# Gate logits taken from the attention's output products, head by head, in a one-core kernel of attention and two expert layers

## The chip, the core and the metric

The kernel runs on one core of a Trainium2 chip. The metric is device time in microseconds of one execution, lower is better; the profile of one execution gives every instruction's start and length. Five engines work side by side: PE (matrix products, with its weight loads shown as PEld), DVE (vector), ACT (activation), POOL, and SP, which here only issues DMAs. Each runs its own list of instructions in order and waits on semaphores.

## What is computed

Three layers follow each other (2 batches, 8 heads, 768 positions, head size 64):

```
q_assign, k_assign = argmax cosine with 16 centroids per head
scores = q k^T / 8, masked where q_assign != k_assign
attn   = softmax(scores) v                              # per batch and head
x      = attn as 1536 tokens x 512 (8 heads x 64)
logits = x @ w_gate                                     # 1536 x 8
tokens go to the 8 experts greedily by descending logit, 192 to each
h      = relu(x[mask] @ w1[e]) @ w2[e]
out    = sum over 4 experts of p[:, e] * relu(h @ v1[e]) @ v2[e]
```

## The kernel before, in words

**Attention** runs over 16 pairs (head, batch), numbered n = 2h + b, in a software pipeline. A "turn" works on pair n (now), n + 1 (soon) and n + 2 (later) at once, and the order of the work of each engine in a turn is written out by hand (the functions `turn` of `block.scalar`, `block.vector` and `block.tensor`). Turns of heads 1 to 6 run in a hardware loop, 12 turns in all; the others are unrolled. Each turn ends two half outputs (u = 0, 1), of three 128-row tiles each.

A half output goes like this. PE multiplies v with the probabilities (`values`, L1334 and L1335). The rows of v are kept as a high and a low part beside each other, so the result `ps_o` has 128 partitions: 64 of the high part, 64 of the low part, by 384 positions. ACT copies it to `oT` (`take_oT`, L716). PE turns it back, three transposes with the identity (`tr_out`, L1353), into the shared bank `ps_m`: 128 positions by 128 columns, high and low beside each other. ACT copies the low columns to `o_low` (`take_low`, L724). DVE adds high and low into `o_sum` (L993) and multiplies by the reciprocal of the softmax sum into `X` (L997, `rows_out`). That product counts up `x_done`, and PE's next use of `ps_m`, the transposes of q and k rows for the later pair (`tr_rows`, L1267), waits for it (L1256, L1264).

**Gate.** After the last of 32 half outputs PE goes through the 12 token tiles (L1397 to L1411): four transposes of `X` with the identity (L1402), ACT copies the result to `xT_tile` (L768), four products of it with `gate_w` (128 columns, of which 8 hold the gate's weights, L1409) into bank 2 of `ps_y`. DVE copies the logits of all tiles (L1046). At the same time SP stores `X` to DRAM in one DMA (L394, 3 MB, 12 KB in a row for each partition and batch); its semaphore is `x_stored`.

**Routing.** Eight phases choose an expert each by a search over the bits of the best logits: DVE compares (L1103), PE counts (L1515), DVE decides. The first phases have no other PE work; `keep_running` (L1501) sends products of no use, to keep PE going. From the end of phase 1 on, PE's expert products (`products`, L1442 and L1457) fill the waits. When an expert's tokens are known, POOL gathers their rows from DRAM (`expert_rows`, L581; before the first it waits for `x_stored`, L604), and SP loads the expert's weights (`expert_weights`, L402 and L405).

**Second layer.** 16 rounds of Strassen-like products in split precision, with their weights loaded by L431 and L438.

**Order of the queues around the change.** SP: centroids (L354), gate weights (L356, after a wait for DVE's clearing of `gate_w`), q, k, v of the first two pairs (L362), `domain_probs` (L379), then the loads and moves of every pair; after them the store of `X`, the store of the normalized `domain_probs` (L420) and the experts' weights. DVE: clears (L898), centroid norms (from L910; they wait for both small loads), attention, the normalization of `domain_probs` (L1040 to L1043), the logits.

## Time and profile before

| what | value |
|---|---|
| median of 3 runs | 1087.37 us (1085.91 to 1087.64) |
| the profiled execution's own time | 1086.81 us |
| its span, first to last instruction | 1085.0 us |
| PE busy | 1024.5 us, 94% of the span |
| DVE busy | 623.0 us, 57% |
| ACT busy | 506.3 us, 47% |
| POOL busy | 441.9 us, 41% |

How to read it: busy shares are averages over stages with different limits, so a change in one stage is read from that stage's own rows. In the view of the instructions in order, a row gives start, length, engine, line, operation, output and inputs, and in brackets how long the engine had been idle and what ended it. Matmuls are pipelined: a row's length is more than its share of PE, and the pace is the distance of starts. The chain is the chain of work that ended last, followed back: each of its pieces holds up the end. A granted clock of 1.00 is PE's full 2.4 GHz, 0.50 is 1.2 GHz.

### The profile page before, as it was taken

What the parts mean: (1) busy time and instruction counts of PE and PEld (TensorE: products, weight loads), DVE (VectorE), ACT (ScalarE), POOL (GpSimd) and SP (SyncE); (2) the same over time, 40 slices, a digit from 0 to 9 for tenths busy, and PEclk for the clock granted to TensorE, in tenths of its full rate; (3) what the DMA queues carried; (4) which work ended last, traced back from release to release, by engine and by line L of the source; (5) the groups of instructions that cost most, each with busy time, mean ns of one, the idle gap of its engine ahead of it and who ended that gap; (6) DMA issues with size and microseconds to landing.
All of it is one profiled execution on the core that took longest, in us unless ns stands there. A gap on an engine that the chain in (4) does not pass through costs nothing.

```text
span 1085.0 us, 18093 instructions
## 1 busy us (share of the span) xinstructions
PE 1024.5 (94%) x6458; PEld 934.0 (86%) x6458; DVE 623.0 (57%) x1332; ACT 506.3 (47%) x1007; POOL 441.9 (41%) x363
## 2 busy tenths in 40 slices
PE   3999999999987799999999999999999999999996
PEld 3888888888877789999899988899999888999995
DVE  2788888888835535555223444555559445555542
ACT  3798888888851233333643333233324332333230
POOL 7032323233100111111266685665566756665542
PEclk9999999999997599999999999999999999999999
DMA  3323232332120724445962212211222322212201
GB/s 97 81 74 82 73 80 75 78 81 71 29 118 14 249 79 170 171 171 171 252 167 78 68 49 78 79 61 60 75 78 70 106 78 79 65 59 72 78 1 59
DMA packets 75170, 99.61 MB, mean 92 GB/s; under 512 B 5728, under 2 KB 44640, under 8 KB 74848
## 3 DMA queue, kind: packets, MB, share of 16 engines
q1 hardware_dynamic: 72400, 92.39, 28.0%
q0 software_dynamic: 2704, 6.33, 1.9%
q8 instruction: 43, 0.70, 0.3%
q14 instruction: 23, 0.19, 0.1%
HBM read 79.80 MB, written 6.32 MB: 79 GB/s over the span
## 4 chain that ended last, share of the span: by engine, by line
PE 83%; ACT 9%; DVE 3%; issue 3%; DMA 1%; POOL 1%; ACTq 0%; SPq 0%; DVEq 0%; POOLq 0%
PE ps_y L1416 9%; PE ps_y L1417 9%; PE ps_y L1415 9%; PE ps_h L1442 8%; PE ps_y L1457 7%; PE ps_h L1417 6%; PE ps_h L1415 6%; PE ps_h L1416 6%; PE ps_t L1320 4%; PE ps_s L1307 3%; ACT p_hi L707 2%; PE ps_s L1308 2%; PE ps_m L1281 2%; PE ps_o L1334 2%; PE ps_o L1335 2%
## 5 line engine op out<-in xcount | busy, mean ns | idle before, releaser
L560 POOL TENSOR_TENSOR w_lo<-w_sum,w_hi 128x1792 fp32r<-128x1792 f32 x32 | 129.8, 4079 | 62.8 <-ACT w_hi L782 62.8
L1417 PE MATMUL ps_y<-b_lo,h_hi 128*128 128x512 f32 x384 | 149.7, 390 | 0.0
L1416 PE MATMUL ps_y<-b_hi,h_lo 128*128 128x512 f32 x384 | 149.7, 390 | 0.0
L1415 PE MATMUL ps_y<-b_hi,h_hi 128*128 128x512 f32 x384 | 149.4, 389 | 0.0
L1231 DVE SCALAR_TENSOR_TENSOR Y<-ps_y,mix_n,Y 128x512 f32<-128x512 f32 x84 | 63.0, 750 | 134.5 <-PE ps_y L1417 134.4
L1415 PE MATMUL ps_h<-x_hi,w_hi 128*128 128x384 f32 x384 | 128.6, 335 | 0.0
L1417 PE MATMUL ps_h<-x_lo,w_hi 128*128 128x384 f32 x384 | 128.5, 335 | 0.0
L1416 PE MATMUL ps_h<-x_hi,w_lo 128*128 128x384 f32 x384 | 128.4, 334 | 0.0
L566 POOL TENSOR_TENSOR b_lo<-b_raw,b_hi 128x2048 fp32r<-128x2048 f32 x16 | 74.0, 4626 | 114.4 <-ACT b_hi L789 113.7
L975 DVE TENSOR_TENSOR p_lo<-ps_t,p_hi 128x384 fp32r<-128x384 f32 x192 | 101.6, 549 | 22.5 <-ACT p_hi L707 22.3
L581 POOL DMA_INDIRECT rows_in<-x_rows,ids x16 | 16.7, 1044 | 222.9 <-DVE ids L1083 212.7
L707 ACT CAST p_hi<-ps_t 128x384 fp32r<-128x384 f32 x192 | 87.2, 485 | 37.4 <-PE ps_t L1320 36.1
L966 DVE TENSOR_REDUCE neg_max<-ps_s 128x1 f32<-128x768 f32 x96 | 91.5, 953 | 18.0 <-PE ps_s L1308 17.9
L795 ACT COPY c<-ps_h 128x384 f32<-128x384 f32 x32 | 15.3, 478 | 179.7 <-PE ps_h L1417 179.7
L801 ACT ACTIVATE h_hi<-ps_h 128x384 fp32r<-128x384 f32 x96 | 47.2, 493 | 103.6 <-DVE ps_h L1188 103.6
L1320 PE MATMUL ps_t<-ident,probs 128*128 128x128 f32 x576 | 87.3, 279 | 7.8 <-DVE p_lo L975 6.3
L1188 DVE TENSOR_TENSOR c<-ps_h,c 128x384 f32<-128x384 f32 x96 | 53.0, 553 | 66.2 <-PE ps_h L1417 64.6
L694 ACT ACTIVATE probs<-ps_s,neg_max 128x768 f32<-128x768 f32 x96 | 88.0, 916 | 2.8 <-DVE neg_max L966 2.8
L520 POOL TENSOR_TENSOR v_rows<-raw_v,ones_t 128x384 fp32r<-128x384 f32 x16 | 13.3, 832 | 186.5 <-PE ps_o L1335 186.5
L1320 PEld LDWEIGHTS ps_t<-ident,probs 128*128 128x128 f32 x576 | 68.5, 143 | 19.8 <-issue 9.4
L1417 PEld LDWEIGHTS ps_y<-b_lo,h_hi 128*128 128x128 f32 x384 | 72.1, 188 | 15.0
L1416 PEld LDWEIGHTS ps_y<-b_hi,h_lo 128*128 128x128 f32 x384 | 72.1, 188 | 14.7
(201 smaller groups left out, 2343.0 us busy)
## 6 DMA issues: line engine op xcount, KB each, us to landing
w_sum<-in_moe_w_dram SPq DMA_DIRECT2D x64, 256.0 KB, 3.2
b_raw<-in_moe_w_dram SPq DMA_DIRECT2D x16, 1024.0 KB
raw_a<-in_moe_w_dram SPq DMA_DIRECT2D x8, 1024.0 KB, 6.5
raw_b<-in_moe_w_dram SPq DMA_DIRECT2D x8, 1024.0 KB
odd_a<-in_moe_w_dram SPq DMA_DIRECT2D x8, 1024.0 KB, 7.5
odd_b<-in_moe_w_dram SPq DMA_DIRECT2D x8, 1024.0 KB
khhT<-kqT SPq DMA_DIRECT2D x32, 192.0 KB, 3.1
raw_k<-in_k_dram SPq DMA_DIRECT2D x16, 192.0 KB, 2.4
```

What stands on the lines that cost most here:

```text
L560: g.tensor_tensor(w_lo[t][:], w_sum[t][:, 1:8], w_hi[t][:].bitcast(F32), ALU.subtract).then_inc(wlo_done[t], 1)
L566: g.tensor_tensor(b_lo[:], b_raw[:], b_hi[:].bitcast(F32), ALU.subtract).then_inc(blo_done, 1)
L694: s.activation(probs[g % 2][:], ps_s[g % 2][:, :, 0:HC], ACT.Exp, bias=neg_max[:, g % 2:g % 2 + 1], scale=1.0, accum_out=row_sum[:, 2 * b ...
L707: s.copy(p_hi[u][:, a * HALF:(a + 1) * HALF, (g % HALF) * P:(g % HALF + 1) * P], ps_t[:, a, 0:HC].rearrange("p (c m) -> p c m", m=P)).then ...
L966: v_.tensor_reduce(neg_max[:, g % 2:g % 2 + 1], ps_s[g % 2][:, :, 0:HC], AX.XY, ALU.max, negate=True).then_inc(max_ready, 1)
L975: v_.tensor_tensor(p_lo[u][sl], ps_t[:, a, 0:HC].rearrange("p (c m) -> p c m", m=P), p_hi[u][sl].bitcast(F32), ALU.subtract).then_inc(plo_ ...
L1320: mm = t_.transpose(ps_t[:, a, c * P:(c + 1) * P], probs[g % 2][:, kt * P:(kt + 1) * P], ident[:])
L1415: t_.matmul(dst, w_hi, x_hi, start=first, stop=False)
L1416: t_.matmul(dst, w_lo, x_hi, start=False, stop=False)
L1417: return t_.matmul(dst, w_hi, x_lo, start=False, stop=last)
L1442: mm = t_.matmul(ps_h[:, H_BANK[j % 3], 0:CAP], wt[i][:, a, f * P:(f + 1) * P], xe[:, a, :], start=(a == 0), stop=(a == KD - 1))
L1457: mm = t_.matmul(ps_y[:, d // 2, (d % 2) * CAP:(d % 2 + 1) * CAP], wt[i][:, f, d * P:(d + 1) * P], h1[:, i * KF + f, :], start=(i == 0 and ...
```

## The change

The transposes of the half output become products. Their weights operand is the same tile of `oT`; their moving operand is no longer the 128-column identity but `eye_gate[:, h]`, 72 columns: on partitions 0 to 63 and again on 64 to 127 it holds the 64 x 64 identity and beside it the 8 gate columns of head h. The sum over partitions adds the high and low parts and multiplies with the gate's weights in one go. DVE scales all 72 columns straight from `ps_m` into `X`, which now has 576 columns per token. The logits are the sum over heads of the 8 extra columns, two reductions, one per batch. The gate's own stage, the copies of the low part and the additions go. The store of `X` is two DMAs, one per batch, in runs of 64 numbers (256 bytes). The normalization of `domain_probs` moves to DVE's start, the loads of the gate's weights behind those of the first pairs. `c_1` moves in memory, for `X` is longer.

```diff
-        X = sb("X", [P, NT, DM], F32, rows)
+        X = sb("X", [P, NT, H * (D + E)], F32, rows)
...
-        gate_w = sb("gate_w", [P, KD, P], F32)
+        c_1 = [sb(f"c_1{i}", [P, HC], F32) for i in range(2)]
...
+        eye_gate = sb("eye_gate", [P, H, D + E], F32, att)
...
             sp.dma_start(cen[:], centroids.rearrange("h c d -> (h c) d")).then_inc(small_in, 16)
-            sp.wait_ge(zeros_done, 1)
-            sp.dma_start(gate_w[:, :, 0:E], w_gate.rearrange("(a p) e -> p a e", p=P)).then_inc(small_in, 16)
...
             load_head(0, 0)
             load_head(0, 1)
+            for a in range(2):
+                sp.dma_start(eye_gate[a * D:(a + 1) * D, :, D:XC],
+                             w_gate.rearrange("(h d) e -> d h e", d=D)).then_inc(gate_in, 16)
...
-            sp.wait_ge(x_done, NU)
-            sp.dma_start(x_dram.rearrange("(b p j) d -> p b (j d)", p=P, j=TPB),
-                         X[:].rearrange("p (b j) d -> p b (j d)", b=B)).then_inc(x_stored, 16)
+            for b in range(B):
+                sp.wait_ge(x_done, NU - 2 + 2 * b)
+                sp.dma_start(x_dram.rearrange("(b p j) (h d) -> b p (j h) d", p=P, j=TPB, d=D)[b],
+                             X[:, b * TPB:(b + 1) * TPB, :].rearrange("p t (h c) -> p (t h) c", c=XC)[:, :, 0:D]).then_inc(x_stored, 16)
...
-            pool.wait_ge(x_stored, 16)
+            pool.wait_ge(x_stored, 16 * B)
...
-            def take_low(at, u):
...
-                s.copy(o_low[:], ps_m[:, 0:HC].rearrange("p (j m) -> p j m", m=P)[:, :, D:P]).then_inc(low_done, 1)
...
-            for t in range(NT):
-                act.wait_ge(gt_full, t + 1)
-                at_least(act, log_full, t - 1)
-                s.copy(xT_tile[t % 2][:].rearrange("p a m -> p (a m)"), ps_h[:, t % 2, :]).then_inc(gt_copied, 1)
...
-            v_.memset(gate_w[:], 0.0).then_inc(zeros_done, 1)
...
-            dve.wait_ge(small_in, 32)
+            dve.wait_ge(small_in, 16)
...
+            for a in range(2):
+                half = slice(a * D, (a + 1) * D)
+                v_.tensor_copy(eye_gate[half, :, 0:D], spread(ident[half, half], 1, [D, H, D])).then_inc(eye_ready, 1)
+
+            dve.wait_ge(probs_in, 16)
+            mlink(v_.tensor_reduce(mix_s[:], mix[:], AX.X, ALU.add), 1)
...
-                dve.wait_ge(low_done, 2 * n + u + 1)
-                v_.tensor_tensor(o_sum[:], ps_m[:, 0:HC].rearrange("p (j m) -> p j m", m=P)[:, :, 0:D],
-                                 o_low[:], ALU.add).then_inc(x_step, 1)
-                dve.wait_ge(x_step, 4 * n + 3 + u)
+                dve.wait_ge(x_step, 2 * n + 2)
+                dve.wait_ge(bt_full, 2 * n + u + 1)
                 t0 = b * TPB + u * HALF
-                v_.tensor_tensor(X[:, t0:t0 + HALF, bass.ds(h * D, D)], o_sum[:],
-                                 spread(rden[:, u * HALF:(u + 1) * HALF], 2, [P, HALF, D]), ALU.mult).then_inc(x_done, 1)
+                v_.tensor_tensor(X[:, t0:t0 + HALF, bass.ds(h * XC, XC)],
+                                 ps_m[:, 0:HALF * XC].rearrange("p (j c) -> p j c", c=XC),
+                                 spread(rden[:, u * HALF:(u + 1) * HALF], 2, [P, HALF, XC]), ALU.mult).then_inc(x_done, 1)
...
+            def head_sums(b):
+
+                dve.wait_ge(x_done, NU - 2 + 2 * b)
+                ts = slice(b * TPB, (b + 1) * TPB)
+                v_.tensor_reduce(logit[:, ts, :], X[:].rearrange("p t (h c) -> p t c h", c=XC)[:, ts, D:XC, :], AX.X,
+                                 ALU.add).then_inc(r_step, 1)
+
             turn(H - 1, 0)
+            head_sums(0)
             turn(H - 1, 1)
-            dve.wait_ge(log_full, NT)
+            head_sums(1)
...
-            v_.tensor_copy(logit[:], ps_log).then_inc(r_step, 1)
...
+                eye = eye_gate[:].rearrange("p h c -> p (h c)")[:, bass.ds(at[1] * XC, XC)]
                 for j in range(HALF):
-                    mm = t_.transpose(ps_m[:, j * P:(j + 1) * P], oT[:, j * P:(j + 1) * P], ident[:])
+                    mm = t_.matmul(ps_m[:, j * XC:(j + 1) * XC], oT[:, j * P:(j + 1) * P], eye, start=True, stop=True)
                 mm.then_inc(bt_full, 1)
...
             pe.wait_ge(x_done, NU)
-            for t in range(NT + 1):
-                if t < NT:
-                    at_least(pe, gt_copied, t - 1)
-                    for a in range(KD):
-                        mm = t_.transpose(ps_h[:, t % 2, a * P:(a + 1) * P], X[:, t, a * P:(a + 1) * P], ident[:])
-                    mm.then_inc(gt_full, 1)
-                if t > 0:
-                    pe.wait_ge(gt_copied, t)
-
-                    c0 = (t - 1) * E
-                    for a in range(KD):
-                        mm = t_.matmul(ps_y[:, 2, c0:c0 + P], xT_tile[(t - 1) % 2][:, a, :], gate_w[:, a, :],
-                                       start=(a == 0), stop=(a == KD - 1))
-                    mm.then_inc(log_full, 1)
```

## Rows read from the trace of the kernel before

**Rows 1.** The page: PE's granted clock in 40 slices of 27 us.
```profile
PEclk9999999999997599999999999999999999999999
```

**Rows 2.** The chain of work from attention's last transposes to the first routing step.
```profile
312.71 0.33 ACT o_low L724
...
331.03 0.26 DVE best L1088
```

**Rows 3.** Groups by line and form, DVE: count, busy us, mean ns, idle before.
```profile
L934 DVE TENSOR_REDUCE cl<-ps_m 128x192 f32<-128x384 f32 x16 | 8.8, 550 | 10.3 <-PE ps_m L1281 10.1
L993 DVE TENSOR_TENSOR o_sum<-ps_m,o_low 128x192 f32<-128x192 f32 x32 | 11.3, 353 | 4.8 <-ACT o_low L724 2.8
L997 DVE TENSOR_TENSOR X<-o_sum,rden 128x192 f32 x24 | 8.6, 359 | 3.8 <-DVE o_sum L993 2.3
L1088 DVE TENSOR_REDUCE best<-logit 128x12 f32<-128x96 f32 x7 | 1.8, 253 | 0.3
```

**Rows 4.** Instructions in order, PE: transposes, 128-column products, and 32-column products.
```profile
328.16 0.60 PE L1402 MATMUL ps_h<-ident,X 128*128 128x128 f32 x4
328.60 2.00 PE L1409 MATMUL ps_y<-gate_w,xT_tile 128*128 128x128 f32 x16
...
156.67 1.49 PE L1281 MATMUL ps_m<-cenT,kqT 128*128 x12
```

**Rows 5.** The chain in an unrolled turn (first row) and in a looped turn.
```profile
44.11 0.30 PE ps_m L1267 x4
...
114.53 0.41 PE ps_m L1267 x4
...
117.65 0.55 PE ps_m L1353 x3
...
119.78 0.41 PE ps_m L1267 x4
...
135.45 0.55 PE ps_m L1353 x3
```

**Rows 6.** Who waited for whom, 40 to 312 us: total us, times, longest.
```profile
PEld ps_m L1267 <- DVE X L997: 4.3, 22, 0.2
```

**Rows 7.** The chain near attention's end, where DVE carries it.
```profile
291.48 0.36 DVE o_sum L993
```

**Rows 8.** The kernel's start: SP's issues in order, then a piece of the chain.
```profile
1.44 0.39 SPq L356 DMA_DIRECT2D gate_w<-in_moe_w_gate_dram  x1
1.87 0.51 SPq L362 DMA_DIRECT2D raw_k<-in_k_dram  x1
...
2.89 4.17 DMA raw_v<-in_v_dram
```

**Rows 9.** DMA issues: count, KB each, median us from issue to landing.
```profile
x_rows<-X SPq DMA_DIRECT2D x1, 3072.0 KB, 8.9
w_sum<-in_moe_w_dram SPq DMA_DIRECT2D x64, 256.0 KB, 3.2
b_raw<-in_moe_w_dram SPq DMA_DIRECT2D x16, 1024.0 KB
```

**Rows 10.** Stages: PE, PEld, DVE, ACT, POOL busy us (count), granted clock, DMA share, GB/s.
```profile
316.00:317.00 1.00, 1.00 (x12) 1.00 (x11) 0.00 (x0) 0.17 (x1) 0.00 (x0) 1.00 0.95 393
336.00:340.00 4.00, 2.45 (x36) 2.03 (x33) 3.07 (x5) 0.00 (x0) 0.00 (x0) 0.63 0.03 6
375.00:380.00 5.00, 5.00 (x25) 4.83 (x24) 3.24 (x13) 2.04 (x7) 0.00 (x0) 0.70 1.05 398
760.00:1000.00 240.00, 240.00 (x1216) 218.53 (x1216) 136.72 (x228) 80.30 (x110) 147.34 (x93) 1.00 0.24 76
```

**Rows 11.** Instructions in order: third from last product into X, first gather, first use of it.
```profile
306.65 0.36 DVE L997 TENSOR_TENSOR X<-o_sum,rden 128x192 f32<-128x192 f32 x1
...
359.94 1.15 POOL L581 DMA_INDIRECT rows_in<-x_rows,ids  x1 [72.36 <-DVE ids L1083]
...
369.68 0.58 PE L1426 MATMUL ps_h<-ident,rows_in 96*128 96x96 f32 x2 [1.79 <-DMA rows_in<-x_rows,ids]
```

More of the change, by code:

```diff
@@ L137, in clustered_attention_two_moes @@
         oT = sb("oT", [P, HC], F32, att)
-        o_low = sb("o_low", [P, HALF, D], F32, att)
-        o_sum = sb("o_sum", [P, HALF, D], F32, att)
         den = sb("den", [P, TPB], F32, att)
         rden = sb("rden", [P, TPB], F32, att)
-        xT_tile = [sb(f"xT_tile{i}", [P, KD, P], F32, att) for i in range(2)]
         att.close()
@@ L165, in clustered_attention_two_moes @@
         sums = ExitStack()
-        c_1 = [sb(f"c_1{i}", [P, HC], F32, sums) for i in range(2)]
         c_16 = [sb(f"c_16{i}", [P, HC], F32, sums) for i in range(2)]
@@ L228, in clustered_attention_two_moes @@
         ps_rt = ps_y[:, 3, :]
-        ps_log = ps_y[:, 2, 0:NT * E].rearrange("p (t e) -> p t e", e=E)
+        XC = D + E
         const_ready = sem("const_ready")
@@ L265, in clustered_attention_two_moes @@
         x_stored = sem("x_stored")
-        gt_full = sem("gt_full")
-        gt_copied = sem("gt_copied")
-        log_full = sem("log_full")
+        gate_in = sem("gate_in")
+        eye_ready = sem("eye_ready")
         r_step = sem("r_step")
@@ L716, in take_oT @@
                 s.copy(oT[:], ps_o[:, 0:HC]).then_inc(oT_done, 1)
-            def take_low(at, u):
-                if not live(at):
-                    return
-                U = 2 * at[0] + u
-                act.wait_ge(bt_full, U + 1)
-                at_least(act, x_done, U)
-                s.copy(o_low[:], ps_m[:, 0:HC].rearrange("p (j m) -> p j m", m=P)[:, :, D:P]).then_inc(low_done, 1)
             def turn(h, b):
@@ L735, in turn @@
                 exp_tile(soon, 1)
-                take_low(now, 0)
                 hi_half(soon, 0, 1)
@@ L752, in turn @@
                 exp_tile(soon, 5)
-                take_low(now, 1)
                 hi_half(soon, 4, 1)
@@ L833, in y_out @@
                 if m == 0:
-                    act.wait_ge(x_stored, 16)
+                    act.wait_ge(x_stored, 16 * B)
                 r = m % 2 * CAP
@@ L921, in _ @@
             dve.wait_ge(const_ready, 10)
-            dve.wait_ge(zeros_done, 2)
+            dve.wait_ge(zeros_done, 1)
             dve.wait_ge(cen_hi, 1)
@@ L925, in _, with mlink @@
                              cenT[:, :, 0, :].bitcast(F32), ALU.subtract).then_inc(cen_lo, 1)
+            for a in range(2):
+                half = slice(a * D, (a + 1) * D)
+                v_.tensor_copy(eye_gate[half, :, 0:D], spread(ident[half, half], 1, [D, H, D])).then_inc(eye_ready, 1)
+            def mlink(ins, i):
+                ins.then_inc(mix_step, 1)
+                dve.wait_ge(mix_step, i)
+            dve.wait_ge(probs_in, 16)
+            mlink(v_.tensor_reduce(mix_s[:], mix[:], AX.X, ALU.add), 1)
+            mlink(v_.tensor_scalar(mix_r[:], mix_s[:], 1e-9, None, ALU.add), 2)
+            mlink(v_.reciprocal(mix_s[:], mix_r[:]), 3)
+            mlink(v_.tensor_tensor(mix_n[:], mix[:], spread(mix_s[:], 2, [P, NT, E2]), ALU.mult), 4)
             shape = [P, 2 * TPB, C]
@@ L984, in row_scale @@
                                  ALU.add).then_inc(x_step, 1)
[L985 removed]
+                dve.wait_ge(x_step, 2 * n + 1)
                 v_.reciprocal(rden[:], den[:]).then_inc(x_step, 1)
@@ L1388, in _ @@
             for n in range(-2, 2):
+                if n == 0:
+                    pe.wait_ge(gate_in, 32)
+                    pe.wait_ge(eye_ready, 2)
                 turn(n // 2, n % 2)
```

14 lines of the change are left out of this document (2 added, 12 removed).

## The prediction

> **What bounds the kernel now.** I read the chain of work first. It has the gate's stage entirely on it: from ACT's copy of the last low part at 312.71 us it goes over DVE's product into X to PE's transposes and products for the gate, and reaches the first routing step at 331.03 [rows 2]. Nothing else can go on meanwhile, because routing needs all logits. In attention the chain is mostly PE's, handed to ACT and back twice a turn; a looped turn takes 135.45 - 117.65 = 17.80 us [rows 5]. The clock view shows one dip, near 340 to 380 us [rows 1], which lies in the early routing phases. Behind them PE is full to the end: 240.00 us busy of 240 [rows 10]. So time taken off before PE's dense work should move everything behind it earlier by as much, unless something new is late.
>
> **The gate's stage.** From 312.71, when the last half output stands in PSUM, to 331.03, when the first routing step starts, are 18.32 us [rows 2]. In its place stand:
> - the product straight from PSUM, 216 columns. The addition that reads PSUM takes 0.353 us for 192 [rows 3]; 24 columns more at about 1 ns each make 0.38.
> - a semaphore step, 0.05.
> - the reduction of the second batch, 384 numbers in. Two prices: the cluster reduction, also of 384 numbers, takes 0.550; the reduction of 96 takes 0.253 [rows 3], and 288 more at 1 ns give 0.54. I take 0.55. It reads with a stride of 288 bytes, for which there is no row; 0.8 is my upper end.
> - the two small clears and the wait behind them, 0.1.
>
> That is 1.1 us, so this part gives **-17.2** (-17.0 to -17.2). The reduction of the first batch costs nothing: it stands in DVE's list behind the 31st product, where DVE had only to wait for PE. The 48 transposes, 96 products (with the doubled last group) and 12 ACT copies need no pricing of their own, as the stage is counted whole.
>
> **The products in place of the transposes** (96 of each). Transposes of fp32 start (0.60 - 0.27)/3 = 0.110 us apart, 128-column fp32 products (2.00 - 0.28)/15 = 0.115, 32-column products (1.49 - 0.26)/11 = 0.112 [rows 4], where 0.26 to 0.28 is the length of a single one. The number of columns makes no difference below 128: something else, the load of 128 weights, sets the pace. 72 columns lie between 32 and 128, so 0.112 to 0.115 against 0.110: +0.2 to +0.5 us over the kernel, not a saving. I take **+0.2**.
> The Trainium skill (FP8 and Floating Point Precision, TensorE Precision Notes) says that true fp32 takes four passes through the array; by an estimate from that, 72 columns would take 4 x 72 / 2.4 GHz = 0.120 us, and the term would be +1.0 us. The trace disagrees: by that rule 128 columns would take 0.213, and they take 0.115, so I keep the row's price.
>
> **Attention, looped turns** (12). The two ACT copies of the low part and the two DVE additions go, but none of them is on the chain there; what they did was make X late. PE's transposes of the next rows wait for X, 4.3 us in 22 waits [rows 6], and on the chain they take 0.41 where an unrolled turn, in which X came in time, shows 0.30 [rows 5]. Without copy and addition X comes about 0.5 us sooner, so both waits should go: 2 x 0.11 x 12 = **-2.6**; the shorter copy list of ACT may bring forward what follows it, which I price at 0. Bounds: 0, if what costs 0.11 is the loop's own address and semaphore work; and -10.2 us, if ACT set the pace of all 16 turns and gave back its two copies (32 x 0.32, the copy's length being [rows 2] 0.33). I take the row's own gap. What is late next: PE's wait for ACT's copies of k and q, which nothing here touches.
>
> **Attention's last two turns.** Here DVE carries the chain and the addition is on it once a half output [rows 7]. Two of them save 0.36 each plus a gap of about 0.1, less 0.02 for the wider product: up to -0.9. I take half, **-0.4**, because PE's and ACT's work is close behind.
>
> **The start.** SP no longer waits for DVE's clear, nor issues the gate's load ahead of q, k, v. The loads of the first pair start at 1.87 [rows 8] and would start at about 1.2, the time at which SP is free of the centroids; their landing is on the chain (2.89 + 4.17, [rows 8]). **-0.7**. The centroid chain starts earlier too. The two identity copies (about 0.5 us each by the rows of DVE above) and the moved normalization, which took 0.9 us under the gate's stage, now go into DVE's ten idle microseconds before its first cluster sums, which hide them. The wait for `domain_probs` in that place has only those sums queued behind it, and the load, issued near 5 us, lands some 6 us before they are due. If that cover fails, attention starts later by what is missing, at most 1 us. SP's two gate loads, 0.4 us of issue each, stand ahead of moves due at 12 us: nothing.
>
> **The store.** The first half is issued when the 30th product is done, at 306.65 + 0.36 = 307.0, the second at the end; POOL needs both at 359.94 [rows 11], which becomes 342.7 after the gate's 17.2. In between are 35.7 us. What has to go through: 12288 pieces of 256 bytes, 768 for each of 16 engines, in place of rows of 12 KB. Large pieces run at 393 GB/s with 0.95 of 16 engines busy, 25.9 bytes per ns and engine; the second layer's loads, half of their bytes in pieces of 512 B, half of 2 KB (64 x 256 KB and 16 x 1024 KB, [rows 9]), at 76 GB/s with 0.24, 19.8 [rows 10]. If the 2 KB pieces go at 25.9, those of 512 B take 32 ns each. A 256 B piece then costs 16 to 32 ns, and the store 12 to 25 us: hidden, with 10 us to spare at the worse end. The old store landed 8.9 us after its issue [rows 9] and was hidden as well. POOL, ACT and SP have nothing queued behind these waits before that time. I take 0.
> The Trainium skill (DMA: Bandwidth & Descriptors, Specifications) says that below 512 bytes a piece needs a read-modify-write. No row here has such pieces in number; this rule speaks against the change and is weighed as a rival below.
>
> **The clock.** It falls near 337 and rises near 378 [rows 10]. With the gate's dense products gone it should fall right at the start of routing. I price that at 0: `keep_running` was paced to be shorter than DVE's comparison even at half clock (30 and 18 small products against comparisons of 1.8 us), so a slower PE there only fills its own waits. The rise hangs on the dense work that starts with the first gather [rows 11], which moves with the rest.
>
> **Sum.** -17.2 + 0.2 - 2.6 - 0.4 - 0.7 = -20.7 us. From the profiled execution's own 1086.8 us: **1066.1 us**. That execution stands 0.6 us below the median of the runs; I leave the number as it is.
>
> **Rivals.**
> - *Attention gives nothing* (0.11 is the loop's own cost): -17.7 us, 1069.1. For it: looped turns pay for addresses in registers everywhere. Against: the wait for X is in the list of waits. 15%.
> - *ACT or DVE set attention's pace*: 1066.1 - (10.2 - 2.6) = 1058.5. For it: both have long lists of work in a turn. Against: the chain's ACT pieces have no copy of the low part among them. 6%.
> - *The clock stays low for longer*: dense work at half clock loses half of its time; 10 us more of it cost 5, 1071. For it: PE loses 17 us of dense work ahead of routing. 8%.
> - *The store is late.* If read-modify-write makes a 256 B piece cost twice one of 512 B, 64 ns, the two halves take 49 us from 307, and need about 1.3 more to land; POOL waits 49.2 + 1.3 - 35.7 = 14.8 us, and PE's first expert product with it: 1081. By the skill's rule this would happen. Against: 512 B pieces at 32 ns leave a factor of 1.4 before the wait starts, at 45 ns. 6%.
> - *Slower than before*: the same mechanism at a higher price. It eats the whole gain when POOL waits over 20.7 us, from (34.4 + 20.7) / 768 = 72 ns a piece; at 100 ns POOL is 42 us late, 1109. Place: POOL's wait for `x_stored` ahead of the first gather. 2%.
>
> **How the numbers follow.** The forecast itself has 63%. Its own range is 1063 to 1068, from the bounds of the start, the reduction and the last turns. The range 1060 to 1073 adds the first and third rivals and part of the second, and leaves out the store's two and the far end of ACT's, some 15%. A measurement of this kernel can tell about 0.2%, 2 us, from no change; only the last rival is slower than that, and a store late by just the gain gives the same: faster 0.97, same 0.01, slower 0.02.
>
> **What would show it.** Right: no gap of more than 2 us between attention's last product and the first routing step; a looped turn of 17.5 to 17.6 us; no wait of L1267 for X; the first q, k, v loads at 1.2 us; both stores landed before POOL's first gather. The products' pace at 0.11. Wrong: POOL's first gather ended by the store instead of by DVE's ids, or a clock row at half speed past the dense products' first 6 us.

## The result, and the profile after

The kernel after takes 1082.77 us, median of 15 runs (1078.31 to 1087.90), beside 1087.70 us for the kernel before in 15 runs of the same session (1083.42 to 1089.84). The ratio is 0.9955, 95% interval 0.9940 to 0.9971: faster by some 5 us. Forecast were 21. The profiled execution of the kernel after took 1083.52 us, its span is 1081.7 us.

The end of attention first, in the chain of work (start, length, what). The first rows are of the kernel before:

```profile
312.12 0.56 PE ps_m L1353 x3
...
327.00 0.44 PE ps_h L1402 x4
327.43 0.89 PE ps_y L1409 x8
...
330.69 0.26 DVE logit L1046
```

and these are those of the kernel after:

```profile
319.95 0.90 PE ps_m L1344 x6
320.95 0.39 DVE X L989
321.36 0.85 DVE logit L1028
322.30 0.26 DVE best L1078
```

The first routing step stood at 331.03 [rows 2] and now stands at 322.30: 8.73 us earlier. Two things of opposite sign make that up. The gate's stage is gone as forecast: from the end of PE's last group to the first routing step were 331.03 - 312.68 = 18.35 us and are 322.30 - 320.85 = 1.45 us. But the group that ends attention now ends at 320.85 instead of 312.68, 8.17 us **later**. Attention became slower.

The counts in these rows say why. The code has three products in the group of L1344 and the chain shows x6; the group of L1353 held three transposes and showed x3. The kernel before already had the same sign in it: for each tile of the gate the code has four transposes (L1402, x4) and four products (L1409, x8). The groups by line, first those of the kernel before:

```profile
L1353 PEld LDWEIGHTS ps_m<-ident,oT x96: 137/140/143, 47.1 to 312.3; 128*128 128x128 f32 x96
L1353 PE MATMUL ps_m<-ident,oT x96: 270/273/332, 47.1 to 312.4; 128*128 128x128 f32 x96
...
L1409 PEld LDWEIGHTS ps_y<-gate_w,xT_tile x96: 186/192/192, 315.2 to 330.2; 128*128 128x128 f32 x96
L1409 PE MATMUL ps_y<-gate_w,xT_tile x96: 275/275/377, 315.2 to 330.3; 128*128 128x128 f32 x96
```

and that of the kernel after:

```profile
L1344 PEld LDWEIGHTS ps_m<-eye_gate,oT x192: 186/192/192, 47.0 to 320.5; 128*128 128x128 f32 x192
L1344 PE MATMUL ps_m<-eye_gate,oT x192: 223/275/330, 47.0 to 320.6; 128*128 x144, 128*128 128x72 f32 x48
```

Columns: instructions, ns min/median/max, first and last start. 96 transposes (16 turns of 6) are 96 instructions. The 96 products in their place are **192**: an fp32 product is two matmul instructions, each with a load of weights of its own. And L1409, which I had read as 96 products at 0.115 us, is 12 tiles of 4, 48 products, so each of them took 0.23.

In the turns this shows as follows, in the chain of the kernel after:

```profile
193.55 0.88 PE ps_m L1344 x6
...
211.81 0.89 PE ps_m L1344 x6
...
230.27 0.88 PE ps_m L1344 x6
```

From 101.57 to 230.27 seven turns take 18.39 us each; they took 17.80 [rows 5]. A group is 0.88 long on the chain where three transposes took 0.55.

The start: the loads of k, q and v go out at 1.20 us instead of 1.87, as forecast, but the landing that the chain waits for is longer (in the chain it starts at 2.13 and takes 4.46, before at 2.89 and 4.17 [rows 8]) and attention's first turn ends only 0.1 us earlier (47.00 against 47.12).

The store, in SP's issues and in the DMA rows of the page:

```profile
313.59 8.31 SPq L391 DMA_DIRECT2D x_rows<-X  x2
321.94 6.26 SPq L417 DMA_DIRECT2D mix_rows<-mix_n  x1
```
```profile
x_rows<-X SPq DMA_DIRECT2D x2, 1536.0 KB, 8.7
```

Its halves go out at 313.6 and 321.4 us and land 8.7 us later; the traffic is over by 330, and POOL gathers first at 350.93. It is hidden. The issue behind it takes 6.26 us, while 6144 pieces are still on their way; in the kernel before the same issue took 0.34. Nothing waits for it.

Now the stage windows (PE, PEld, DVE, ACT, POOL busy us and count, granted clock, DMA share, GB/s) of the kernel after, and below them PE's instructions at the third gather's rows (each expert's rows are gathered from DRAM by two DMAs; I number the gathers by expert):

```profile
325.00:330.00 5.00, 2.49 (x45) 2.05 (x46) 3.78 (x12) 0.00 (x0) 0.00 (x0) 0.75 0.93 212
...
350.00:365.00 15.00, 12.50 (x96) 11.16 (x97) 6.83 (x26) 1.13 (x2) 2.80 (x3) 0.50 0.51 135
365.00:370.00 5.00, 5.00 (x33) 4.95 (x32) 4.32 (x18) 3.11 (x10) 0.00 (x0) 1.00 0.99 375
416.00:418.00 2.00, 0.12 (x1) 0.00 (x0) 0.00 (x0) 0.00 (x0) 0.00 (x0) 1.00 0.00 0
418.00:420.00 2.00, 0.04 (x1) 0.04 (x1) 0.00 (x0) 0.00 (x0) 0.00 (x0) 0.91 0.00 0
420.00:428.00 8.00, 8.00 (x38) 7.09 (x39) 1.50 (x4) 1.61 (x3) 0.00 (x0) 0.50 0.01 2
```
```profile
419.96 1.54 PE L1406 MATMUL ps_h<-ident,rows_in 96*128 96x96 f32 x8 [3.85 <-DMA rows_in<-x_rows,ids]
```

The clock falls in early routing as before, in two stretches: near 337 to 351 and 354 to 378 us in the kernel before (the forecast took them for one), 327 to 342 and 348 to 365 in the kernel after. New is a long one behind the second gather: PE stands for 3.85 us in front of the third gather's rows, and then works at 1.2 GHz (clock 0.50) until about 430. In the kernel before nothing of the kind is there; its third gather was waited for by nobody. From the first routing step to the end of the span the kernel before takes 754.0 us (1085.0 - 331.03), the kernel after 759.4 (1081.7 - 322.30). That gives back 5.4 us. The stretches between the first routing step and the transposes of the second, fourth and eighth gathers' rows show what it is made of, first in the kernel before, then in the kernel after:

```profile
331.03:401.81 70.78, 58.18 (x553) 53.16 (x551) 37.74 (x128) 16.60 (x36) 5.68 (x6) 0.71 0.38 131
401.81:454.54 52.73, 52.52 (x444) 49.21 (x442) 26.79 (x95) 20.41 (x48) 5.71 (x6) 1.00 0.50 176
454.54:558.36 103.82, 101.60 (x806) 95.81 (x805) 44.29 (x141) 46.30 (x103) 22.13 (x23) 1.00 0.64 185
```
```profile
322.30:389.84 67.54, 55.87 (x547) 50.56 (x545) 37.72 (x128) 16.60 (x36) 5.98 (x6) 0.75 0.52 161
389.84:451.40 61.56, 57.41 (x444) 52.92 (x441) 26.80 (x95) 20.49 (x48) 5.71 (x6) 0.92 0.44 150
451.40:555.06 103.66, 101.44 (x804) 95.92 (x805) 44.28 (x141) 46.26 (x103) 22.10 (x23) 1.00 0.65 187
```

Around the third gather 8.8 us are lost (61.56 against 52.73, for the same 444 matmuls). Early routing gives 3.2 us back (67.54 against 70.78), since PE no longer waits for the first gather (1.79 us before [rows 11]) and the clock is low for less long. The rest is the same.

So the miss of the profiled execution, 1083.5 - 1066.1 = 17.4 us, has two parts. The first routing step is 8.73 us earlier where 20.7 were forecast: 12.0. Behind it are the 5.4.

### The profile page after: what moved, and what is told of

Same layout as the page of the kernel before. It is cut to its first block, busy times and chain, and to the rows that moved or that the text cites. A ratio compares the mean times of both kernels' runs of the same rounds, so it can differ in the third digit from the quotient of the medians.

```text
span 1081.7 us, 17912 instructions
## 1 busy us (share of the span) xinstructions
PE 1017.8 (94%) x6410; PEld 932.3 (86%) x6410; DVE 620.5 (57%) x1302; ACT 490.7 (45%) x963; POOL 442.0 (41%) x363
## 4 chain that ended last, share of the span: by engine, by line
PE 80%; ACT 11%; issue 3%; DVE 2%; DMA 2%; POOL 1%; ACTq 0%; SPq 0%; DVEq 0%
PE ps_y L1397 9%; PE ps_y L1396 9%; PE ps_y L1395 9%; PE ps_h L1422 8%; PE ps_y L1437 6%; PE ps_h L1397 6%; PE ps_h L1395 6%; PE ps_h L1396 6%; PE ps_t L1310 4%; ACT probs L691 3%; PE ps_s L1297 3%; ACT p_hi L704 2%; PE ps_m L1344 2%; PE ps_m L1271 2%; PE ps_o L1324 2%
## 5 line engine op out<-in xcount | busy, mean ns | idle before, releaser
L960 DVE TENSOR_REDUCE neg_max<-ps_s 128x1 f32<-128x768 f32 x96 | 91.8, 956 | 18.9 <-PE ps_s L1298 18.5
L1310 PE MATMUL ps_t<-ident,probs 128*128 128x128 f32 x576 | 84.3, 278 | 7.3 <-DVE p_lo L969 6.2
L1395 PEld LDWEIGHTS ps_y<-b_hi,h_hi 128*128 128x128 f32 x384 | 72.1, 188 | 14.6
```

The costliest lines, as they stand in the source:

```text
L960: v_.tensor_reduce(neg_max[:, g % 2:g % 2 + 1], ps_s[g % 2][:, :, 0:HC], AX.XY, ALU.max, negate=True).then_inc(max_ready, 1)
L1310: mm = t_.transpose(ps_t[:, a, c * P:(c + 1) * P], probs[g % 2][:, kt * P:(kt + 1) * P], ident[:])
L1395: t_.matmul(dst, w_hi, x_hi, start=first, stop=False)
```

## The experiments

Each group of kernels ran on one chip with the kernel before beside it, and each ratio is to that. Behind the first three stands **theory A**: the products' two instructions each cost attention what the forecast lacks. Its rival: something else in the change slowed attention (the copies gone from ACT's list, the wider product on DVE). The fourth asks whether time taken off ahead of routing arrives at the end.

### The kernel after once more

No edit.

> The changed kernel once more, unchanged. Theory A (two losses): attention is slower by passes, and a wait for the third gather of rows (3.9 us, with a clock dip behind it) takes another part of the gain. If that wait belongs to the change, it shows again at the third gather and the ratio to before stays near 0.9955. Rival (chance of one execution): another gather, or none, waits, and the profiled execution then lies near 1075 us. The looped turn is 18.3 to 18.5 us in either case.

Measured: 1084.48 us (1079.37 to 1088.88, 6 runs), ratio 0.9948 (0.9929 to 0.9967). The first ratio stands, and the wait for the third gather shows again. The profiled execution is the longest of the six, span 1087.1, and shows more of the same:

```profile
419.25 1.06 PE L1406 MATMUL ps_h<-ident,rows_in 96*128 96x96 f32 x5 [3.58 <-DMA rows_in<-x_rows,ids]
...
536.23 1.54 PE L1406 MATMUL ps_h<-ident,rows_in 96*128 96x96 f32 x8 [3.88 <-DMA rows_in<-x_rows,ids]
```

Two gathers are late here, the third and the seventh, and 765.0 us pass from its first routing step to its end.

### One pass instead of two

```diff
-        eye_gate = sb("eye_gate", [P, H, D + E], F32, att)
+        eye_gate = sb("eye_gate", [P, H, D + E], F32R, att)
+        eye_raw = sb("eye_raw", [P, H, E], F32, att)
...
-        oT = sb("oT", [P, HC], F32, att)
+        oT = sb("oT", [P, HC], F32R, att)
...
+            dve.wait_ge(gate_in, 32)
+            v_.tensor_copy(eye_gate[:, :, D:XC], eye_raw[:]).then_inc(eye_ready, 1)
```

> The changed kernel with oT and eye_gate rounded to fp32r, so that each product of the output step is one pass instead of two; this leaves out the low bits of the attention output. Theory A (an fp32 product is two instructions of 0.11 us each on PE): 96 instructions go, a looped turn falls from 18.4 to about 17.5 us, attention ends 12 to 14 us earlier, time near 1070. Rival B (the turn is longer because DVE's product now waits for PE directly, or the exponent's wait moved): the turn stays above 18.1 us and the time above 1079.

Measured: 1079.56 us (1077.41 to 1087.47, 7 runs), ratio 0.9934 (0.9905 to 0.9962); span of the profiled execution 1075.6. Its products and its first routing step:

```profile
L1347 PE MATMUL ps_m<-eye_gate,oT x96: 194/281/303, 46.9 to 310.8; 128*128 x72, 128*128 128x72 f32 x24
```
```profile
312.54 0.25 DVE L1081 TENSOR_REDUCE best<-logit 128x12 f32<-128x96 f32 x1
```

96 products are 96 instructions, and routing starts 9.8 us earlier than in the kernel after, 18.5 earlier than before. A looped turn (103.27 to 227.37, seven turns) takes 17.73 us. The distance to the forecast's start of routing (331.03 - 20.7 = 310.3) is 2.2 us now. The count, the turn and the start of routing are those of theory A, though attention gained 9.8 us where 12 to 14 were expected. The time is not: 1070 was expected, and 1079.56 lies where the rival had it, only some 7 us below that of before by the ratio. From routing to the end this kernel takes 763.1 us, with waits of 1.13, 4.17, 0.33 and 0.54 us for its first, third, fourth and seventh gathers. What attention gave is lost behind it.

### The products alone, in the kernel before

```diff
-                    mm = t_.transpose(ps_m[:, j * P:(j + 1) * P], oT[:, j * P:(j + 1) * P], ident[:])
+                    mm = t_.matmul(ps_m[:, j * P:(j + 1) * P], oT[:, j * P:(j + 1) * P], ident[:], start=True, stop=True)
```

> The kernel before with one part of the change alone: products with the 128-column identity in place of the three transposes of each half output; all else as before. Theory A: each becomes two instructions, the turn grows from 17.8 to 18.3 to 18.4 us, time plus 9 us, near 1096. Rival B: products cost PE what transposes cost, the turn stays at 17.8 and the time within 1.5 us of before.

Measured: 1098.20 us (1096.83 to 1099.69, 5 runs), ratio 1.0088 (1.0072 to 1.0103), that is +9.6 us; the first routing step at 338.78, 7.75 us later than before. A looped turn takes 18.37 us.

```profile
L1353 PE MATMUL ps_m<-ident,oT x192: 270/275/378, 46.1 to 320.1; 128*128 128x128 f32 x192
```

96 more instructions at the transposes' pace of 0.110 are 10.6 us; 7.75 of them show at the first routing step, and the rest of the 9.6 stands behind it. Theory A is shown from both sides: nothing of the rest of the change is in this kernel, and attention becomes slower all the same.

### Without the gate's stage

The kernel before, with the transposes, products and copies of the stage left out; the logits are a sum over some of X's columns.

> The kernel before without the gate's stage; the logits are left out and replaced by a reduction over columns of X, attention as before. My forecast's main term: 17.2 us less, 1.1 of them given back because the normalization of domain_probs now lies open, so near 1071.5 if all behind moves along. Rival C (the routing and expert stage takes part of any gain back, whatever attention does): 1075 to 1079, with a wait for a gather of rows or a longer stretch at half clock in the profile. Turn 17.8 us.

Measured: 1074.60 us (1072.95 to 1075.77, 4 runs), ratio 0.9864 (0.9845 to 0.9882): -14.8 us by the ratio, where 16.1 were expected and some 9 to 13 by rival C. The first routing step is 15.0 us earlier (316.02; the mix's normalization and a reduction of 1.43 us stand exposed in this kernel). So most of the time that is taken off ahead of routing does arrive at the end. How much is lost on the way a single profile can't say: from routing to the end this one takes 758.0 us, beside 754.0 in the kernel before, but the kernel before with small pieces stored (below) takes 758.6 with its gate's stage in place. No gather from the second on was waited for by more than 0.4 us.

### Whose is the late gather?

Three profiles of kernels with the new attention show the third gather late, three without it do not. The moment in the span is not what decides: the gather's second DMA is issued at 412.00 and 411.56 us in the two profiles of the kernel after, where it is late, and at 411.86 in the next kernel below, where it is in time. **Theory S**: the store in 256-byte pieces does it. I tried it both ways.

```diff
-                sp.dma_start(x_dram.rearrange("(b p j) (h d) -> b p (j h) d", p=P, j=TPB, d=D)[b],
-                             X[:, b * TPB:(b + 1) * TPB, :].rearrange("p t (h c) -> p (t h) c", c=XC)[:, :, 0:D]).then_inc(x_stored, 16)
+                sp.dma_start(x_dram.rearrange("(b p j) d -> b p (j d)", p=P, j=TPB)[b],
+                             X[:, b * TPB:(b + 1) * TPB, :].rearrange("p t c -> p (t c)")[:, 0:TPB * DM]).then_inc(x_stored, 16)
```

> The kernel after, with both stores of X written as whole stretches of each partition instead of 256-byte pieces (it copies the first 3072 columns of each half as they lie, so the rows stored are not the attention's rows in order; later stages read other numbers). Three profiles of kernels with the new store show the wait for the third gather (3.85, 3.58, 4.17 us), three of kernels with the old store show none. Theory S, the pieces are what makes that gather's landing late: no wait for the third gather, its transposes about 4 us after the gather's second issue, and the whole about 8 us below the kernel after, a ratio near 0.987 to before. Rival R, the pieces have nothing to do with it (another part of the change, or the shift of everything by some 10 us): the wait of 3.6 to 4.2 us stands, ratio 0.995 as before.

Measured: 1083.44 us beside 1091.98, ratio 0.9925 (0.9900 to 0.9949), where theory S wanted 0.987 and its rival 0.995. The profiled execution (span 1077.3) has no wait for the third gather, as theory S wants, and one of 0.91 for the fourth. But it is the fastest of the six executions, with a mean granted clock of 0.978; four of the others took 1083.3 to 1084.9 us at 0.974, so the clock was low for longer in them. They may hold a late gather that this profile does not show.

```diff
-            sp.wait_ge(x_done, NU)
-            sp.dma_start(x_dram.rearrange("(b p j) d -> p b (j d)", p=P, j=TPB),
-                         X[:].rearrange("p (b j) d -> p b (j d)", b=B)).then_inc(x_stored, 16)
+            for b in range(B):
+                sp.wait_ge(x_done, NU - 2 + 2 * b)
+                for h in range(H):
+                    hs = slice(h * D, (h + 1) * D)
+                    sp.dma_start(x_dram.rearrange("(b p j) d -> b p j d", p=P, j=TPB)[b][:, :, hs],
+                                 X[:, b * TPB:(b + 1) * TPB, hs]).then_inc(x_stored, 16)
```

> The kernel before, with X stored in 256-byte pieces (one transfer for each head and half of the tokens, behind the same semaphore), nothing else changed. Theory S: the third gather lands late here too, a wait of about 4 us in front of its transposes and with the half clock behind it about 8 us more, ratio near 1.007. Rival R: no wait at the third gather, ratio 0.999 to 1.001. A store that is slow in itself would show as a first gather later than 359.9 us.

Measured: ratio 0.9995 (0.9974 to 1.0015), third gather in time. Small pieces cost the kernel before nothing and do not make its gather late. So the pieces alone are not the cause. That they help to it in the new kernel is not excluded: the ratio with large pieces lies between the two expectations.

### More slack for the gathers

The kernel issues a gather's second DMA 3.95 us before PE comes to its rows. **Theory G**: in some executions the landing takes longer than that, and an earlier issue gives the time back.

```diff
-                    products(fill[2 * i])
-                    keep_running(warm[2 * i])
-                    if i == 1 and n > 0:
+                    if i == 1 and n > 1:
+                        products(fill[2] - 6)
                         slot_tokens(n - 1)
+                        products(6)
+                    else:
+                        products(fill[2 * i])
+                        keep_running(warm[2 * i])
+                        if i == 1 and n > 0:
+                            slot_tokens(n - 1)
```

> The kernel after, with the slot tokens' products of phases 2 and on put 6 units (12 products, 2.1 us) ahead of where they stand, so that every gather from the second or third on is issued 2.1 us earlier against the product stream that waits for it. Theory G (the gather's landing takes up to 8 us from its second issue in some executions, and the kernel leaves it 3.95 us): the wait shrinks from 3.9 to about 1.8 us where it shows, and the time falls 2 to 5 us below the kernel after, ratio 0.991 to 0.994. Rival: the landing is late by whatever is next in line, so that the gather issued earlier lands at the same moment, or no gather is late in the executions timed: ratio 0.995 as without the edit. The 12 products put behind the slot tokens may hold up the next digit's count by up to 2 us a phase on VectorE, which would give back some.

> The same edit in the kernel before. No gather from the third on was waited for in its profile, so theory G says there is nothing to gain: ratio 0.998 to 1.001. If it gains 3 us or more, late gathers are part of the kernel before too, in the executions that were not profiled; if it loses, the later count of the next digit costs, and that loss has to be added to what e7 shows.

Measured: 1082.09 us, ratio 0.9913 (0.9884 to 0.9942) in the kernel after, 1.0013 (0.9995 to 1.0031) in the kernel before. The third gather is late in this profile too, and now costs 1.42 us, with no fall of the clock behind it:

```profile
419.91 0.88 PE L1406 MATMUL ps_h<-ident,rows_in 96*128 96x96 f32 x8 [1.42 <-DMA rows_in<-x_rows,ids]
```

That fits theory G: where the third gather is late, its rows are released 7.6 to 8.3 us behind the second issue, in this kernel as in the three above, and PE now comes 6 us behind it instead of 4. The kernel before has nothing to gain. The interval of 0.9913 reaches into that of the first kernel, so the ratio alone decides nothing.

### What makes a gather late

In the kernel after POOL issues the third gather like this:

```profile
410.73 0.96 POOL L578 DMA_INDIRECT rows_in<-x_rows,ids  x1 [28.52 <-DVE ids L1073]
412.00 1.19 POOL L578 DMA_INDIRECT rows_in<-x_rows,ids  x1 [0.30 <-issue]
413.19 0.69 POOL L585 DMA_DIRECT2D slot_token<-ids  x1
```

The traffic around it:

```profile
412.00:415.00 3.00, 3.00 (x28) 2.52 (x27) 1.02 (x5) 0.00 (x0) 1.88 (x2) 1.00 0.46 131
415.00:420.00 5.00, 1.15 (x8) 0.86 (x7) 0.89 (x1) 0.00 (x0) 0.00 (x0) 0.96 0.00 0
```

No rows move from 415 on, yet PE is released at 419.96. So the rows had been moved and only their completion was missing. Right behind the gather, on the same queue, goes the slot tokens' transfer: 96 pieces of 4 bytes to DRAM, which by the page takes 8.0 us from issue to landing (here 8.4). **Theory K**: a gather is late when its last completions fall behind that transfer's writes. The Trainium skill (DMA: Bandwidth & Descriptors, Anatomy of one DMA) has a sentence that fits: a semaphore is raised only when the write is confirmed, and "This can cause a surprisingly long delay especially when the write target is HBM." The 8 us for 384 bytes fit it, though no run here takes the confirmation apart from the rest. Whether such a write also holds up the gather ahead of it is what the next runs try.

```diff
                 expert_rows(n)
+                if n < E - 1:
+                    pool.wait_ge(xt_full, n + 1)
                 keep_ids(n)
```

> The kernel after, with the transfer of the slot tokens to DRAM (96 pieces of 4 bytes, issued 1.2 us behind the second issue of every gather) held back until the gathered rows are transposed. In the profiles the rows of every gather have moved some 3 us after the second issue, but its last landings come up to 8 us after it in some, and the slot tokens' transfer, whose own landings take 8 to 10 us, is under way just then. Theory K, that transfer is what makes a gather late: no wait over 0.5 us in front of any gathered rows' transposes, the third 3.95 us behind its second issue, and the time 3 to 5 us below the kernel after: ratio 0.987 to 0.991. Rival: the landing is late by something else (the shift by 9 us, the layout): the wait of 3.6 to 4.2 us stays in the profile, ratio 0.995.

> The same edit in the kernel before. Its profiles show a wait of 1.8 to 3.7 us for the first gather and none for the third. Theory K: the first wait goes, 1.5 to 3 us in all, ratio 0.997 to 0.999, the first transposes 6.3 us behind the second issue (another wait, for PE's own work, ends there). Rival: nothing moves, ratio 1.000.

> The kernel with one-pass products (as in the run with them before) and the slot tokens' transfer held back: the two causes that the study names for the forecast's error taken away together. Its routing should start at 312.5 us as before, and if the rest costs the 754 to 758 us that it costs where no gather is late, the span is 1067 to 1070 and the ratio 0.981 to 0.984: the forecast's 1066 plus the wait for the first gather. Rival: the rest is as long as it was with one pass (763 us), ratio 0.993: then what the shorter attention gains is lost behind it for a cause not yet named.

Measured, beside 1091.05 us for the kernel before: 1084.16 us, ratio 0.9928 (0.9904 to 0.9952); in the kernel before 1094.53, 1.0035 (1.0013 to 1.0058), **slower**; with one pass 1076.12, 0.9858 (0.9824 to 0.9892). The times missed the expectations. The traces went by the theory: no wait is left for the first gather (1.79 us in the kernel before [rows 11]) and none over 0.5 us for the third, in three profiles of three; only the kernel before waits 1.26 us for its sixth, whose rows themselves move later there. The transfer that is held back takes 8.6 us by itself. In the run on the kernel after:

```profile
358.67 1.54 PE L1410 MATMUL ps_h<-ident,rows_in 96*128 96x96 f32 x8
389.77 0.82 PE L1410 MATMUL ps_h<-ident,rows_in 96*128 96x96 f32 x8
415.89 0.82 PE L1410 MATMUL ps_h<-ident,rows_in 96*128 96x96 f32 x8
```

The eighth transposes stand 225.9 us behind the first routing step (232.8 in the kernel after), but the rest then takes 535.5 us instead of 526.6. The waits from 545 to 570 us show by what:

```profile
POOL ids_all L590 <- DMA slot_token<-ids: 9.1, 1, 9.1
ACT w_hi L768 <- POOL w_sum L552: 8.6, 2, 7.9
...
PE ps_y L1441 <- ACT h L799: 5.9, 2, 4.7
```

My edit held back the seventh transfer as well. It now stood in front of the domain mix's rows, POOL came late to the weights' sums, ACT waited for POOL with h behind it in its list, and PE for ACT. So the edit was cut down to the first six gathers:

```diff
-                if n < E - 1:
+                if n < EARLY:
```

> The kernel after, with the slot tokens' transfer held back for the first six gathers only. In the run that held back all, every gather landed in time and the first routing step and the eighth transposes stood 225.9 us apart (232.8 in the kernel after), but the rest took 535.5 us instead of 526.6, since the seventh transfer now stood in front of the domain mix's rows and POOL came 4.6 us late to the weights' sums. If both readings hold, the rest is 526 to 529 us again: span 1074 to 1077, ratio 0.986 to 0.989, 6 to 9 us below the kernel after. Rival: the transposes stay in time and the rest stays at 535 us, ratio 0.993: then the loss behind the eighth gather has another cause.

> One-pass products and the transfer held back for the first six gathers. Routing from 311.7 to 312.5 us, the eighth transposes 226 to 228 us behind it, the rest 526 to 529: span 1064 to 1069, ratio 0.977 to 0.981, the forecast's 1066 in the profiled run. Rival as in the run before this one: the rest stays at 534 us, ratio 0.986.

> The same six transfers held back in the kernel before, whose first gather was waited for 1.8 to 3.7 us in five profiles. Its rest behind the eighth gather should be 526 to 529 us again instead of 537.8, and its first wait gone: ratio 0.996 to 0.999. If it stays at 1.003, the edit costs this kernel something by itself (the transfer behind the transposes meets the weights' loads) and that cost must be in the two runs beside it too.

Measured, beside 1090.77 us for the kernel before:

| kernel | median us | ratio | span | routing at | routing to end |
|---|---|---|---|---|---|
| after, six held back | 1078.55 | 0.9885 (0.9860 to 0.9911) | 1074.2 | 321.59 | 752.6 |
| one pass, six held back | 1070.58 | 0.9817 (0.9791 to 0.9844) | 1067.1 | 311.79 | 755.3 |
| before, six held back | 1089.46 | 0.9987 (0.9972 to 1.0003) | 1088.4 | 329.47 | 758.9 |

The ratios are those that were expected (one pass a trace above, its interval reaches in), and so are the spans of the first two. Behind the eighth transposes these take 527.2 and 527.6 us, as expected; the kernel before takes 532.3, some 3 us more than was expected of it. That need not be the edit's doing: with small pieces and with the earlier gathers, both without it, the kernel before takes 531.2 and 530.9 there. The third gather's wait and the second dip of the clock are gone (kernel after with six held back):

```profile
415.00 0.88 PE L1410 MATMUL ps_h<-ident,rows_in 96*128 96x96 f32 x8 [0.41 <-DMA rows_in<-x_rows,ids]
```
```profile
416.00:420.00 4.00, 4.00 (x33) 3.36 (x31) 1.50 (x4) 1.43 (x3) 0.69 (x1) 1.00 0.06 4
420.00:428.00 8.00, 8.00 (x59) 7.61 (x59) 5.48 (x26) 3.81 (x12) 0.00 (x0) 1.00 0.22 19
```

Compare the last row with that of the kernel after above: the same 8 us hold 59 matmuls at 2.4 GHz instead of 38 at 1.2. The edit is worth 0.7% in the kernel after (0.9885, interval 0.9860 to 0.9911, against 0.9955 and 0.9948, of which the lowest end is 0.9929) and 0.1%, within its interval, in the kernel before. That is what theory K asks for: with the transfer out of the way the waits and the time go. Two things it does not settle. The edit moves the transfer's issue on POOL as well as its writes, and no run takes these apart, so that the completions fall behind the writes is argued, not shown. And a gather can be late with nothing behind it on its queue. In the kernel before with six held back the sixth is:

```profile
505.68 0.88 PE L1430 MATMUL ps_h<-ident,rows_in 96*128 96x96 f32 x8 [1.44 <-DMA rows_in<-x_rows,ids]
```

The second kernel of the table is the fastest of the study, 20 us below before; its products take their inputs as fp32r, so it buys part of that with precision.

## Why the prediction was wrong

The sign was right, the size was not: 1066.1 us with 1060 to 1073 forecast, 1082.8 measured.

- **The gate's stage, -17.2: right.** It went from 18.35 to 1.45 us, -16.9. What is missing is the strided reduction: 0.85 us, where I took 0.55 and had 0.8 as the upper end.
- **The products in place of the transposes, +0.2 to +0.5: this step failed.** Alone it measured +7.75 us at the first routing step and +9.6 us in the time, against 10.6 by 96 more instructions at 0.110. I priced a product by the distance between two *instructions* of L1409 and never counted them against the code. 2.00 us for "x16" [rows 4] is 8 products. My words "96 products (with the doubled last group)" explained the count of 96 away instead of asking why 12 tiles of 4 should give it. The sentence "by that rule 128 columns would take 0.213, and they take 0.115" compared the four passes of the Trainium skill (FP8 and Floating Point Precision, TensorE Precision Notes) with half a product; a whole one takes 0.22 to 0.23, near the estimate for 128 columns. For 72 columns the trace disagrees: the estimate's 0.120 would have made a product hardly dearer than a transpose, and a turn takes as long with 72 columns as with 128 (18.39 us in the kernel after, 18.37 with the products alone). So the nearness at 128 may be chance. That part of the step, no gain from fewer columns, was right.
- **Looped turns, -2.6: right in kind, too large.** PE's wait of L1267 for X [rows 6] is gone from the list of waits, and those transposes take 0.29 to 0.30 us on the chain. But with one pass a turn takes 17.73 us, not 17.5 to 17.6: 0.07 us less than before instead of 0.22, over 12 turns -0.8 us instead of -2.6. What took the place of the wait was not tried. The list of waits has a new one that may be it: before the weights of the products the weight loads stand idle 4.8 us in all, in nine times, for nothing that the profile shows (1.0 us, twice, in the kernel before). The doubled products then add what makes a turn 18.39.
- **Last two turns, -0.4, and start, -0.7: too large.** The loads did go out 0.67 us earlier, but 0.1 us of it was left at 47 us. Both together are under a microsecond of the miss.
- **The store, 0: right.** Both halves landed 20 us ahead of the first gather. Storing in small pieces alone gave a ratio of 0.9995. The rule of the Trainium skill (DMA: Bandwidth & Descriptors, Specifications), read-modify-write below 512 bytes, costs this kernel no time: the store runs at 212 to 233 GB/s, somewhat over half of the 393 of large pieces, and 6144 pieces landed in 8.7 us. Whether a read-modify-write is what lowers the rate no run shows, and that it doubles a piece's cost was my own assumption.
- **The clock, 0, and "a shift moves everything behind it": wrong in the kernel after.** Most of a shift does arrive (-15.0 at routing gave a time 14.8 us lower without the stage). What I did not see is that the kernel gives a gather 3.95 us between its second issue and its rows' first use, and that its completion may take 8. After a wait of 3.6 to 4.2 us there the clock was at 1.2 GHz for 7 to 10 us. In the profile of the kernel after the two cost 8.8 us; 3.2 us that early routing gained make it the 5.4. One pair of profiles is a weak measure of that, because from routing to the end the profiles of kernels with the old attention (no transfer held back) range from 754.0 to 760.8 us, though the third gather is in time in all of them. The better one is the held-back transfers: 0.7% in the kernel after, some 7 us, and 0.1% in the kernel before.
- **The rivals.** None of the five is what happened. The nearest was "the clock stays low for longer", which I priced without naming a wait that would cause it.

Nearly the whole distance is accounted for: with one pass and the six transfers held back the profiled execution takes 1068.94 us (its span is 1067.1) and the ratio is 0.9817, beside 1066.1 and 0.9804 (1066.1 / 1087.37) forecast. Part of that nearness is luck. That kernel also saves the wait for the first gather, which the forecast did not count on: it needs 68.6 us from the first routing step to the second gather's rows where the kernel before needed 70.8.

**What stays open.** Why the third gather is late in four profiles of five with the new attention, and in none of five without it (those with the transfers held back left aside), was not found. The store's pieces alone do not decide it, nor the point in time; the layout of SBUF and the order in which 4-byte writes and completions meet were not tried by themselves. With the old attention the same transfer stands behind the third gather, and that gather is in time. Held-back transfers left no wait over 0.41 us there in four profiles of four with the new attention, which names the partner in the collision but not its mechanism.

## What to carry to other kernels

Before a duration is taken from a group of matmuls, divide its count by the number in the code: an fp32 product is two instructions and a transpose is one, so replacing transposes by products doubled their time here even where it added nothing else. Ask of every transfer that is needed within a few microseconds what is issued behind it on its queue; small writes to DRAM whose result is needed much later belong behind the moment of use, but no further: held back in front of the domain mix's rows, the seventh cost 9 us here. And when a part of a profile moves, the end is not moved by the same amount until the waits that had no slack to spare have been looked at one by one: here 4 us of lateness cost nearly 9, as the clock fell with it.

## What the runs showed that was not expected

- An fp32 product is two instructions at 72 columns as at 128, with weight loads of 192 ns against 140 for a transpose; with fp32r inputs it is one instruction.
- 96 pieces of 4 bytes to DRAM take 8 to 9 us to land, and with them behind it a gather was completed 5 us after its rows had moved. With them out of the way no first gather was waited for, and no third for over 0.5 us, in six profiles; of the ten others, seven show a wait of 1.0 to 3.7 us for the first gather. A sixth gather was still waited for by 1.3 and 1.4 us in two of the six.
- Such lateness probably makes much of the scatter too: the kernel after ran from 1078 to 1088 us (15 runs), and with six transfers held back from 1076.0 to 1078.9 (6 runs); with one pass from 1077.4 to 1087.5 (7 runs), and with six held back from 1068.4 to 1072.6 (6 runs).
- An issue on SP behind 6144 small pieces took 6.26 us, behind the large pieces of the kernel before 0.34.
